# Second products of both tiles in one stretch, and earlier combinations of x and w, in a seven-product feed-forward kernel

## The chip, the cores and the metric

One core of one Trainium2 chip (trn2) runs the kernel. The metric is the device time in microseconds of one execution. The kernel before took 927.95 us (median of 3 runs, 927.69 to 928.31). A measurement of this kernel can tell about 0.2% (1.9 us) from no change.

## The reference

Three stages on 4 x 576 = 2304 tokens, all in float32:

```
scores = softmax(q k^T / 8) in chunks of 64 tokens, 8 heads of 64   # attention
x = scores v                                                        # 2304 x 512
y = ((x @ w_a) * (x @ w_b)) @ w_out                                 # 512 -> 1536 -> 512
h = y @ w_in;  g = P(h) / (Q(h) + 1e-6);  out = g @ w_out2          # 512 -> 2048 -> 512
```

P is a cubic with coefficients a, and Q = 1 + |b0||h| + |b1|h^2.

## The kernel before, in words

Every float32 product is made as three TensorE products of rounded halves (hi x hi, hi x lo, lo x hi). So each operand is first rounded to a "hi" part (a cast on ScalarE, `round_...`), and the rest is subtracted to a "lo" part (on GpSimd or VectorE, `rest_...`). All five engines run hand-written queues that meet at semaphores; an engine does its instructions strictly in the order in which they are written.

**Attention, merged with the first products.** 18 units of 128 tokens go through a pipeline (turns of 3 units), and between its steps TensorE does `merged_block`: the first two of twelve feature groups (`G1` = 2, the "first weights", cut into pieces by `FIRST_CUTS`) for five of the six tiles of 384 tokens. The sixth tile follows (`first1`, `second1(PLAIN)` and `second1(PLAIN + 1)`, L603 and L620).

**The quads.** The other ten feature groups of the middle stage are done two tiles at a time (3 pairs of tiles, 10 "quads" each, 30 in all). A quad n computes a 2 x 2 block product (two halves of the 512 inputs; the two tiles; the columns of w_a and w_b of one feature group) with seven products in place of eight. `quad_head(n)` (L649) does three of them, A11, S3 and S2; `quad_tail(n)` (L667) does A12, S1, A22 and S4. Each is 6 matmuls of 384 columns (`seven`, issued at L637). A11, A12 and A22 are blocks of the weights, S1 to S4 combinations that GpSimd makes (`sums`, L406), ScalarE rounds (`round_w`, L857) and GpSimd completes (`rest_ws`, L424). The other side needs combinations of x: T1, T2, T3 and T4, once per pair of tiles, of 128 x 768 each (`make_t1`, `make_t2`, `make_t4`, `round_t`, `rest_t`). GpSimd makes those of pair 0 during attention, VectorE those of pairs 1 and 2 between its other work.

**Around a quad.** ScalarE copies a product's bank as the seed of the next (`seed`, L926, which `quad_head` awaits before S2) and takes two partial results out (`copy_p7`, L931, and `copy_u2`, L936). VectorE's `corners(n)` (L1138 to L1145) adds and multiplies four times; the last matmuls of the quad, S4, wait for its first instruction (`c22_done`, L1138), which itself needs S1 to be done. The two results, one for each tile, are the gated values g of this feature group: ScalarE rounds them (`round_g`, L946), VectorE makes the rest (`rest_g`, L1150).

**A block** (`blk`, 15 in all) is quads 2 blk and 2 blk + 1, and between their parts the second products of the block before: `second_sum(blk - 1, ti)` for tile ti = 0 and 1, 24 matmuls each (L590), whose four banks VectorE adds to y (`add_y`, L1128). They need `wo_ready` (`round_wo`, L865, and `rest_wo`, L429). `round_g(n, ti)` waits for the `second_sum` of the same ti, since that still reads the older g. In block 0 there is no `second_sum`; `second1(PLAIN + 1)` of 12 matmuls (L626) stands in its place.

**Where weights lie.** `w` has four slots. Even quads use W_EVEN, odd ones W_ODD; the raw weights of even quads from 2 on come through a staging area. Part of the first weights lies in the columns S4 and up of W_ODD, so quad 1's combinations cannot be made before these are used up (`out_done`).

**The last stage** is 32 steps m of `first2(m)` (24 matmuls) and `second2(m - 3)` (18), with a rational function on ScalarE and VectorE in between. `second2(1)` needs the four pieces of its weights; the last piece is loaded after the last `second_sum`, rounded by ScalarE at step 3 (`round_w2(1, PPF2 - 1)`, L870) and completed by GpSimd (`rest_w2`, L434).

Of the kernel before, what the change touches and what calls it, by code (L numbers as in the profile page):

```python
# [20 lines left out]
def attention_moe_moe2(nc, q, k, v, w_a, w_b, w_out1, w_in, w_out2, a, b, out):  # L21
# [21 lines left out]
    PW = 512  # L43
# [41 lines left out]
    with ExitStack() as ctx:  # L85
# [118 lines left out]
        def first_w(half, start, n):  # L204
            if start < SLOT:
                assert start + n <= SLOT
                return w[:, T_ODD, half, start:start + n]
            return w[:, W_ODD, half, S4 + start - SLOT:S4 + start - SLOT + n]

        FIRST_CUTS = (0, PW, 2 * PW, 3 * PW, 4 * PW, SLOT, PPG1 * PW)  # L210
# [42 lines left out]
        LEAD_SPLIT = {2: (0, 1), 3: (2, 3), 4: (4, 5)}  # L253
        X2_AT = {2 * BPP: 0, 2 * BPP + 1: 1, 2 * BPP + 2: 2, 2 * BPP + 3: 3}

        def order_of_sums(n):
            return {0: 0, 1: 2, 2: 1}.get(n, n - 1 if n % 2 == 0 else n + 1 if n + 1 < QUADS else n)
# [31 lines left out]
        def _(sp):  # L289
# [53 lines left out]
            load_ab(0)  # L343
            load_wo(0)
            load_ab(1)
# [7 lines left out]
            load_wo(2)  # L353
            for blk in range(BLOCKS):
                if blk > 0:
                    sp.wait_ge(p3_done, 2 * blk)
                    load_ab(2 * blk + 1)
                    sp.wait_ge(sum_done1, DC * 2 * blk)
                else:
                    sp.wait_ge(out_done, G1)  # L360
                load_wo(2 * blk + 1)
                if 2 * blk + 4 < QUADS:
                    sp.wait_ge(ws_ready, 3 * (2 * blk + 3))
                    load_ab(2 * blk + 4)
                if 0 < blk < BLOCKS - 1:
                    sp.wait_ge(wo_ready, 2 * blk + 1)
                    load_wo(2 * blk + 2)
                if blk == 2 * BPP:
                    sp.wait_ge(p3_done, 2 * QPP)
                    for i in range(PPF2):  # L370
                        load_w2(0, i)
# [19 lines left out]
        def _(pool):  # L391
# [14 lines left out]
            def sums(n):  # L406

                pool.wait_ge(ab_loaded[n % 2], 32 * (n // 2 + 1))
                if n == 1:
                    pool.wait_ge(out_done, G1)  # L410
                half = lambda at: raw_w(n, at, at + HALF)
                nc.gpsimd.tensor_tensor(half(S1), half(S3), half(A22), ALU.add).then_inc(s1_done, 1)
                pool.wait_ge(s1_done, order_of_sums(n) + 1)
                nc.gpsimd.tensor_tensor(half(S2), half(S1), half(A11), ALU.subtract).then_inc(s2_done, 1)
                nc.gpsimd.tensor_tensor(half(S3), half(A11), half(S3), ALU.subtract).then_inc(sums_done, 1)
                pool.wait_ge(s2_done, order_of_sums(n) + 1)
                nc.gpsimd.tensor_tensor(half(S4), half(A12), half(S2), ALU.subtract).then_inc(sums_done, 1)
# [47 lines left out]
            for i in range(PPG1):  # L465
                rest_first(i)
# [34 lines left out]
        def _(pe):  # L501
# [186 lines left out]
            def merged_block(t, r, last=False):  # L688
# [12 lines left out]
                else:  # L701
                    pe.wait_ge(w_ready, PPG1)
# [100 lines left out]
        def _(act):  # L803
            def attention(turn, slot, stages):
                i = turn * RING + slot

                def split_first():
                    for n in LEAD_SPLIT.get(i, ()):
                        at, to = FIRST_CUTS[n], FIRST_CUTS[n + 1]
                        act.wait_ge(raw1_loaded[n], 16)  # L810
                        nc.scalar.copy(first_w(HI, at, to - at), y_flat[:, at:to]).then_inc(w_hi_done, 1)
# [47 lines left out]
            def round_wo(n):  # L859
                act.wait_ge(wo_loaded[n % 2], 16 * (n // 2 + 1))  # L860
                if n == 1:
                    act.wait_ge(out_done, G1)
                elif n >= 2:
                    act.wait_ge(sum_done1, DC * 2 * (n // 2))
                nc.scalar.copy(w[:, w_slot(n), HI, WO:SLOT], raw_w(n, WO, SLOT)).then_inc(wo_hi_done, 1)  # L865
# [6 lines left out]
            def round_t(pair, i):  # L872
                raw, hi, lo = t_parts(pair, i)
                act.wait_ge(t_made, T_MAKES * pair + (T_MAKES if i == T4 else 6))
# [82 lines left out]
            for blk in range(BLOCKS):  # L957
# [16 lines left out]
                round_w(n + 1, 1)  # L974
                round_w(n + 1, 2)
# [10 lines left out]
                if blk > 0:  # L986
                    round_wo(n)
# [17 lines left out]
            for m in range(STEPS2 + LAG2):  # L1005
# [50 lines left out]
        def _(dve):  # L1056
# [103 lines left out]
            def make_t1(pair):  # L1160
# [7 lines left out]
                nc.vector.tensor_tensor(t1, raw, x_block(x_hi, pair, 0, 0), ALU.subtract).then_inc(t_made, 1)  # L1168
                dve.wait_ge(t_made, made + 2)
                nc.vector.tensor_tensor(t1, t1, x_block(x_lo, pair, 0, 0), ALU.subtract).then_inc(t_made, 1)  # L1170

            def make_t2(pair):
                made, raw, (t1, t2, t4) = T_MAKES * pair, x_raw(pair), t_raw(pair)
                nc.vector.tensor_tensor(t4, x_block(x_hi, pair, 1, 1), x_block(x_lo, pair, 1, 1), ALU.add).then_inc(t_made, 1)
# [18 lines left out]
            for blk in range(BLOCKS):  # L1193
                n = 2 * blk
                if blk == 0:
# [4 lines left out]
                corners(n)  # L1200
# [4 lines left out]
                pair, part = blk // BPP + 1, blk % BPP  # L1205
# [97 lines left out]
```

## Time and profile before

| | |
|---|---|
| median of 3 runs | 927.95 us |
| the profiled execution, its own time | 927.83 us |
| its span | 926.1 us |
| TensorE busy | 903.2 us (98%) |
| VectorE busy | 676.3 us (73%) |
| ScalarE busy | 515.5 us (56%) |
| GpSimd busy | 361.4 us (39%) |
| mean granted TensorE clock | 0.996 of full |
| stages, from the chain of waits | attention to 158 us, quads to 512 us, last stage to the end |

The span is shorter than the time of the execution by 1.7 us, which lies around it. In the rows further on, a stretch is from:to in us from the span's start; a row of the chain is start, duration, engine, what it writes, line and how many instructions; a row of the timeline gives in brackets how long the engine had been idle before, and what released it.

### The profile page before, as it was taken

To read this page: it belongs to the slowest core of one execution; us is meant where nothing else is said; L and a number is where in the kernel's file an instruction comes from. 1 tells how busy PE (TensorE), PEld (TensorE's weight loads), DVE (VectorE), ACT (ScalarE), POOL (GpSimd) and SP (SyncE) were. 2 spreads that over 40 slices of the span, in tenths; PEclk is the share of its full clock that TensorE was granted. 3 is DMA by queue.
4 is the path that set the end of the run, shared out by engine and by line. 5 is a ranking of instruction groups with operands and counts; after the bars stand their busy time and mean duration, and the time that the engine had idled before them with its cause. 6 is when DMAs were issued, how large, how long until landed. Compare 5 with 4: busy or idle time off the path is not lost.

```text
span 926.1 us, 14075 instructions
## 1 busy us (share of the span) xinstructions
PE 903.2 (98%) x5596; PEld 852.7 (92%) x5596; DVE 676.3 (73%) x874; ACT 515.5 (56%) x786; POOL 361.4 (39%) x301
## 2 busy tenths in 40 slices
PE   8999999899899999999999989999999999999998
PEld 8899999899899999999999989999999999999996
DVE  3656552467655666665664798998999999989987
ACT  4655564333444445445553577776766666665662
POOL 2106133777867777778985223210111001100000
PEclk9999999999999999999999999999999999999999
DMA  9754611122122222123212020002000100000102
GB/s 212 165 104 103 137 24 35 58 69 65 49 69 69 69 69 58 51 73 106 84 53 73 20 91 1 1 1 91 0 1 1 57 35 1 1 1 22 48 35 102
DMA packets 103234, 53.35 MB, mean 58 GB/s; under 512 B 58880, under 2 KB 94720, under 8 KB 103168
## 3 DMA queue, kind: packets, MB, share of 16 engines
q1 hardware_dynamic: 103168, 52.45, 21.3%
q8 instruction: 44, 0.72, 0.3%
q14 instruction: 22, 0.18, 0.1%
HBM read 47.71 MB, written 4.72 MB: 57 GB/s over the span
## 4 chain that ended last, share of the span: by engine, by line
PE 90%; DVE 5%; issue 2%; ACT 1%; POOL 1%; DVEq 0%; ACTq 0%; POOLq 0%
PE ps L590 41%; PE ps L758 21%; PE ps L637 20%; PE ps L509 3%; PE ps L533 2%; PE ps L551 2%; PE ps L505 1%; DVE g_lo L1150 1%; POOL w L424 0%; PE ps L626 0%; DVE w L1168 0%; DVE w L1189 0%; DVE tmp L1138 0%; ACT g_hi L946 0%; DVE tmp L1247 0%
## 5 line engine op out<-in xcount | busy, mean ns | idle before, releaser
L590 PE MATMUL ps<-x_hi,w 128*128 128x384 f32 x960 | 255.3, 337 | 0.2 <-issue 0.2
L758 PE MATMUL ps<-w,g_hi 128*128 128x512 f32 x576 | 177.6, 391 | 2.6 <-POOL w L434 2.6
L590 PEld LDWEIGHTS ps<-x_hi,w 128*128 128x128 f32 x960 | 174.4, 188 | 2.9 <-issue 0.5
L590 PE MATMUL ps<-x_lo,w 128*128 128x384 f32 x480 | 160.8, 335 | 0.0
L590 PE MATMUL ps<-g_hi,w 128*128 128x384 f32 x560 | 148.7, 336 | 0.7 <-issue 0.7
L637 PE MATMUL ps<-x_hi,w 128*128 128x384 f32 x480 | 137.1, 341 | 11.8 <-DVE tmp L1138 8.1
L434 POOL TENSOR_TENSOR w<-w 128x512 fp32r<-128x512 f32 x32 | 46.9, 1470 | 240.5 <-ACT w L870 240.5
L758 PEld LDWEIGHTS ps<-w,g_hi 128*128 128x128 f32 x576 | 107.3, 188 | 23.9 <-POOL w L434 2.9
L758 PE MATMUL ps<-w,g_lo 128*128 128x512 f32 x288 | 112.1, 392 | 0.0
L1128 DVE TENSOR_TENSOR y<-y,ps 128x384 f32<-128x384 f32 x120 | 65.7, 553 | 59.5 <-PE ps L590 59.5
L637 PE MATMUL ps<-w 128*128 128x384 f32 x540 | 103.3, 334 | 0.0
L590 PEld LDWEIGHTS ps<-g_hi,w 128*128 128x128 f32 x560 | 101.7, 188 | 1.5 <-issue 1.1
L637 PEld LDWEIGHTS ps<-x_hi,w 128*128 128x128 f32 x480 | 89.7, 192 | 14.0 <-DVE tmp L1138 10.0
L946 ACT CAST g_hi<-tmp 128x384 fp32r<-128x384 f32 x60 | 30.8, 514 | 117.4 <-DVE tmp L1143 91.6
L637 PEld LDWEIGHTS ps<-w 128*128 128x128 f32 x540 | 94.6, 188 | 0.0
L590 PE MATMUL ps<-g_lo,w 128*128 128x384 f32 x280 | 93.6, 334 | 0.0
L590 PEld LDWEIGHTS ps<-x_lo,w 128*128 128x128 f32 x480 | 90.1, 188 | 1.7
L637 PE MATMUL ps<-x_lo,w 128*128 128x384 f32 x240 | 81.6, 340 | 0.0
L1030 ACT ACTIVATE w<-tmp,bias_ln 128x768 f32<-128x768 f32 x48 | 45.1, 940 | 60.5 <-DVE tmp L1253 60.3
L1013 ACT ACTIVATE tmp<-ps 128x768 f32<-128x768 f32 x48 | 39.0, 812 | 68.5 <-PE ps L590 68.5
L424 POOL TENSOR_TENSOR w<-w 128x512 fp32r<-128x512 f32 (+1 forms) x48 | 70.0, 1488 | 18.0 <-ACT w L857 16.8
L1247 DVE SCALAR_TENSOR_TENSOR tmp<-tmp,coef 128x768 f32<-128x768 f32 x48 | 53.3, 1110 | 30.2 <-ACT tmp L1016 30.1
(113 smaller groups left out, 1593.8 us busy)
## 6 DMA issues: line engine op xcount, KB each, us to landing
w<-in_moe_w_out SPq DMA_DIRECT2D x32, 256.0 KB, 3.5
out<-y SPq DMA_DIRECT2D x18, 256.0 KB, 2.0
y<-in_q SPq DMA_DIRECT2D x16, 256.0 KB, 4.3
y<-in_k SPq DMA_DIRECT2D x16, 256.0 KB, 4.5
y<-in_v SPq DMA_DIRECT2D x16, 256.0 KB, 3.3
w<-in_moe_w_a SPq DMA_DIRECT2D x16, 256.0 KB, 3.0
w<-in_moe_w_b SPq DMA_DIRECT2D x16, 256.0 KB, 3.4
w<-in_moe_w_in SPq DMA_DIRECT2D x16, 256.0 KB, 3.9
```

Source lines behind the costliest of these rows:

```text
L424: nc.gpsimd.tensor_tensor(w[:, w_slot(n), LO, at:to], raw_w(n, at, to), w[:, w_slot(n), HI, at:to], ALU.subtract).then_inc(ws_ready, 1)
L434: nc.gpsimd.tensor_tensor(w2_at(w, fp, LO, i), w2_at(w32, fp, LO, i), w2_at(w, fp, HI, i), ALU.subtract).then_inc(w2_ready, 1)
L509: last = nc.tensor.transpose(ps[:, bank, r * P:(r + 1) * P], x[:, r * P:(r + 1) * P], ident[:])
L533: last = nc.tensor.matmul(ps[rows, SC, at], qT[rows, at], kT[rows, at], start=True, stop=True)
L590: last = nc.tensor.matmul(dst, left, right, start=n == 0, stop=n == 3 * len(pairs) - 1)
L637: last = nc.tensor.matmul(ps[:, bank, 0:TILE], left, moving, start=i == 0 and not onto, stop=i == 5, skip_group_check=onto)
L758: last = nc.tensor.matmul(out_bank(n), left[:, 2 * (m % 2) + e, u * P:(u + 1) * P], w[:, slot2(fp), right, DC * HALF + e * D:DC * HALF + ( ...
L946: nc.scalar.copy(g_hi[:, 2 * ti + n % 2, :], corner[:, 2 * (n % 2) + 1 - ti, :]).then_inc(g_hi_done, 1)
L1013: nc.scalar.activation(habs, h, ACT.Abs).then_inc(habs_done, 1)
L1030: nc.scalar.activation(rec, den3[m % 2], ACT.Ln, scale=2.0 ** -SHIFT, bias=bias_ln[:, 0:1]).then_inc(ln_done, 1)
L1128: nc.vector.tensor_tensor(y[:, t, at], y[:, t, at], ps[:, 4 + c, 0:TILE], ALU.add).then_inc(y_added, 1)
L1247: nc.vector.scalar_tensor_tensor(out=den[cur], in0=den[cur], scalar=coef[:, 6:7], in1=habs, op0=ALU.add, op1=ALU.mult).then_inc(den_done, 1)
```

## The change

- **Order of a block on TensorE.** `quad_head(2 blk)` and `quad_tail(2 blk)` now follow each other, and `second_sum(blk - 1, 0)` and `second_sum(blk - 1, 1)` come behind them in one stretch (in block 0: `second1(PLAIN + 1)`). On VectorE `corners(2 blk)` goes ahead of `add_sums(blk - 1, 0)`.
- **Combinations of x for pairs 1 and 2** are spread over five blocks: two instructions behind `rest_g(n, 1)` in each, and the rests of T1 and T2 at the start of the blocks of parts 3 and 4. Before it was 3, 3, 4 and 2 instructions in the blocks of parts 1 to 4.
- **Quad 1's weights.** The first weights that lay in W_ODD from S4 on now lie in the WO columns of both W slots. So `sums(1)`, `round_w(1, ...)` and `rest_ws(1)` are done during attention, with earlier loads; in exchange the second weights of quads 0 and 1 (`load_wo`, `round_wo`, `rest_wo`) wait for `out_done` in block 0. A piece of the first weights is cut in two.
- **Pair 0** (T1 to T4) and quad 0's weights are rounded one step earlier in attention.
- **Last stage.** `round_w2(1, PPF2 - 1)` moves from the end of step 3 to the end of step 2 on ScalarE.

```diff
-            return w[:, W_ODD, half, S4 + start - SLOT:S4 + start - SLOT + n]
-        FIRST_CUTS = (0, PW, 2 * PW, 3 * PW, 4 * PW, SLOT, PPG1 * PW)
+            slot, at = (W_EVEN, W_ODD)[(start - SLOT) // D], WO + (start - SLOT) % D
+            assert at + n <= SLOT
+            return w[:, slot, half, at:at + n]
+        FIRST_CUTS = (0, PW, 2 * PW, 3 * PW, 4 * PW, SLOT, SLOT + D, PPG1 * PW)
...
@@ SyncE
-            load_ab(0)
-            load_wo(0)
-            load_ab(1)
+                if unit == 10:
+                    load_ab(0)
+                if unit == 12:
+                    load_ab(1)
...
-            load_wo(2)
             for blk in range(BLOCKS):
...
                 else:
                     sp.wait_ge(out_done, G1)
+                    load_wo(0)
                 load_wo(2 * blk + 1)
...
+                if blk == 0:
+                    sp.wait_ge(wo_hi_done, 1)
+                    load_wo(2)
@@ GpSimd
-                if n == 1:
-                    pool.wait_ge(out_done, G1)
...
             sums(0)
+            sums(1)
             for i in T_ORDER:
                 rest_t(0, i)
             rest_ws(0)
-            rest_wo(0)
+            rest_ws(1)
             sums(2)
             for blk in range(BLOCKS):
-                sums(2 * blk + 1)
-                rest_ws(2 * blk + 1)
+                if blk > 0:
+                    sums(2 * blk + 1)
+                    rest_ws(2 * blk + 1)
                 if blk < BLOCKS - 1:
                     rest_ws(2 * blk + 2)
-                if blk > 0:
-                    rest_wo(2 * blk)
+                rest_wo(2 * blk)
                 rest_wo(2 * blk + 1)
@@ TensorE
                 quad_head(2 * blk)
+                quad_tail(2 * blk)
                 if blk == 0:
                     second1(PLAIN + 1)
                 else:
                     second_sum(blk - 1, 0)
-                quad_tail(2 * blk)
-                if blk > 0:
                     second_sum(blk - 1, 1)
@@ ScalarE, attention
-                    if j == 1 and r == 4:
+                    if j == 1 and r == 3:
                         round_t(0, T1)
                         round_t(0, T2)
-                    if j == 1 and r == 5:
+                    if j == 1 and r == 4:
                         round_t(0, T3)
                         round_t(0, T4)
+                    if j == 1 and r == 5:
+                        round_w(0, 0)
+                        round_w(0, 1)
...
-                round_w(0, r)
-                if r == 2:
-                    round_wo(0)
+                if r == 0:
+                    round_w(0, 2)
+                round_w(1, r)
@@ ScalarE, blocks
-                round_w(n + 1, 0)
+                if blk > 0:
+                    round_w(n + 1, 0)
                 pair, part = blk // BPP + 1, blk % BPP
+                if pair < PAIRS and part == 2:
+                    round_t(pair, T1)
                 if pair < PAIRS and part == 3:
-                    round_t(pair, T1)
...
+                if m == 2:
+                    round_w2(1, PPF2 - 1)
                 if m == 3:
-                    round_w2(1, PPF2 - 1)
@@ VectorE
+                if pair < PAIRS:
+                    if part == 3:
+                        rest_t(pair, T1)
+                    if part == 4:
+                        rest_t(pair, T2)
+                corners(n)
                 if blk == 0:
                     for c in range(DC):
                         add_y(TILES - 1, -1, c)
                 else:
                     add_sums(blk - 1, 0)
-                corners(n)
                 rest_g(n, 0)
...
+                    if part == 0:
+                        make_t1_first(pair)
                     if part == 1:
-                        make_t1(pair)
+                        make_t1_last(pair)
                     if part == 2:
                         make_t2(pair)
                     if part == 3:
                         make_t4(pair)
-                        rest_t(pair, T1)
-                        rest_t(pair, T2)
```

The last instruction of `make_t1` and the first of `make_t2` are `make_t1_last`. Two places show how the instructions move.

VectorE in block 1, before, from `rest_g(2, 1)` to quad 3's first `corners` instruction (L1166 to L1170 are `make_t1` of pair 1):

```order
L1150 TENSOR_TENSOR g_lo<-tmp,g_hi 128x384 [waits g_hi_done]
L1166 TENSOR_TENSOR x_lo<-x_hi,x_lo 128x2x384 [waits out_done]
L1168 TENSOR_TENSOR w<-x_lo,x_hi 128x768 [waits t_made]
L1170 TENSOR_TENSOR w<-w,x_lo 128x768 [waits t_made]
L1138 TENSOR_TENSOR tmp<-ps,tmp 128x384 [waits p7_copied,p5_done]
```

The same engine after the change, from the end of quad 0's `corners` in block 0 to quad 1's first `corners` instruction (L1137 is `add_y`, L1161 `rest_g`, L1177 and L1179 `make_t1_first` of pair 1, L1149 the first of `corners`):

```order
L1156 TENSOR_TENSOR tmp<-ps,tmp 128x384 [waits p3_done]
L1137 COPY y<-ps 128x384 [waits out_done] x4
L1161 TENSOR_TENSOR g_lo<-tmp,g_hi 128x384 [waits g_hi_done] x2
L1177 TENSOR_TENSOR x_lo<-x_hi,x_lo 128x2x384 [waits out_done]
L1179 TENSOR_TENSOR w<-x_lo,x_hi 128x768 [waits t_made]
L1149 TENSOR_TENSOR tmp<-ps,tmp 128x384 [waits p7_copied,p5_done]
```

In block 1 one of the three instructions between `rest_g` and `corners` is gone; block 0, which had none there, has two.

ScalarE in block 0 after the change, from `copy_u2(0)` to `copy_u2(1)` (L954 is `round_g(0, ...)`, L862 `round_w(2, ...)`, L934 `seed(1)`, L870 `round_wo(0)`):

```order
L944 COPY tmp<-ps 128x384 [waits g_ready,p6_done]
L954 CAST g_hi<-tmp 128x384 [waits out_done,prod1_done]
L862 CAST w<-tmp 128x512 [waits p3_done,ab_loaded_even]
L862 CAST w<-tmp 128x512 [waits sums_done]
L862 CAST w<-tmp 128x768 [waits sums_done]
L954 CAST g_hi<-tmp 128x384 [waits out_done,prod2_done]
L934 COPY ps<-ps 128x384 [waits prod2_done,p1_done]
L870 CAST w<-w 128x512 [waits out_done,wo_loaded_even]
L939 COPY tmp<-ps 128x384 [waits g_ready,p7_done]
L944 COPY tmp<-ps 128x384 [waits g_ready,p6_done]
```

The three casts of quad 1's weights are gone from behind `copy_u2(0)`, and a cast of quad 0's second weights now stands between `seed(1)` and the copies of quad 1.

## Rows read from the trace of the kernel before

**Rows 1.** The page: busy times, and the chain that ended last by engine.

```profile
PE 903.2 (98%) x5596; PEld 852.7 (92%) x5596; DVE 676.3 (73%) x874; ACT 515.5 (56%) x786; POOL 361.4 (39%) x301
...
PE 90%; DVE 5%; issue 2%; ACT 1%; POOL 1%; DVEq 0%; ACTq 0%; POOLq 0%
```

**Rows 2.** Waits of TensorE: us in total, times, longest.

```profile
PE ps L637 <- DVE tmp L1138: 8.1, 6, 2.4
PE ps L637 <- POOL w L424: 3.7, 1, 3.7
PE ps L758 <- POOL w L434: 2.6, 1, 2.6
```

**Rows 3.** Stretches by block: length, busy PE, PEld, DVE, ACT, POOL; then clock.

```profile
158.18:183.46 25.28, 21.63 (x116) 21.31 (x115) 10.58 (x17) 9.72 (x19) 16.53 (x15) 0.93 0.17 52
183.46:207.59 24.13, 23.16 (x134) 22.84 (x133) 16.41 (x23) 9.63 (x18) 18.78 (x17) 1.00 0.24 67
...
231.72:258.81 27.09, 24.72 (x133) 24.40 (x133) 17.53 (x24) 11.83 (x21) 19.44 (x17) 0.94 0.22 60
258.81:281.69 22.88, 22.88 (x133) 22.88 (x133) 14.38 (x22) 10.27 (x19) 17.85 (x16) 1.00 0.22 64
...
352.83:377.83 25.00, 23.16 (x134) 22.84 (x133) 17.32 (x24) 11.84 (x21) 18.32 (x16) 1.00 0.26 72
```

**Rows 4.** The chain that ended last, in blocks 1 to 4.

```profile
202.56 0.56 DVE tmp L1138
...
203.16 4.43 PE ps L637 x24
...
252.82 5.99 PE ps L637 x24
...
271.29 10.40 PE ps L637 x60
```

**Rows 5.** Timeline of VectorE in block 1.

```profile
197.76 0.94 DVE L1166 TENSOR_TENSOR x_lo<-x_hi,x_lo 128x768 f32<-128x768 f32 x1
198.74 1.93 DVE L1168 TENSOR_TENSOR w<-x_lo,x_hi 128x768 f32<-128x768 f32 x1
```

**Rows 6.** Timeline of GpSimd in block 1.

```profile
193.07 4.35 POOL L424 TENSOR_TENSOR w<-tmp,w 128x512 fp32r<-128x512 f32 x3 [1.65 <-ACT w L857]
198.09 1.75 POOL L429 TENSOR_TENSOR w<-tmp,w 128x512 fp32r<-128x512 f32 x1 [0.67 <-ACT w L865]
```

**Rows 7.** The chain that ended last: block 0, and the start of the last stage.

```profile
166.54 4.61 POOL w L424 x3
...
171.20 12.26 PE ps L637 x60
...
548.38 4.38 PE ps L758 x18
```

**Rows 8.** Timeline of ScalarE in block 1.

```profile
192.38 1.88 ACT L857 CAST w<-tmp 128x512 fp32r<-128x512 f32 x3
...
197.02 0.46 ACT L926 COPY ps<-ps 128x384 f32<-128x384 f32 x1 [0.47 <-PE ps L637]
```

**Rows 9.** DMA issues by kind: KB each, median us from issue to landing.

```profile
w<-in_moe_w_out SPq DMA_DIRECT2D x32, 256.0 KB, 3.5
```

**Rows 10.** Timelines of GpSimd, TensorE and VectorE in the last stage.

```profile
546.79 1.53 POOL L434 TENSOR_TENSOR w<-w 128x512 fp32r<-128x512 f32 x1 [31.23 <-ACT w L870]
...
548.38 0.73 PE L758 MATMUL ps<-w,g_hi 128*128 128x512 f32 x2 [2.59 <-POOL w L434]
...
574.25 1.00 DVE L1266 SCALAR_TENSOR_TENSOR tmp<-tmp,coef,ps 128x768 f32<-128x768 f32 x1
```

**Rows 11.** Timelines of ScalarE and VectorE near the end of attention.

```profile
134.27 0.61 ACT L857 CAST w<-w 128x512 fp32r<-128x512 f32 x1
134.79 0.58 ACT L835 CAST x_hi<-ps 128x512 fp32r<-128x512 f32 x1
...
140.34 0.56 DVE L1100 TENSOR_TENSOR tmp<-ps,tmp 128x384 f32<-128x384 f32 x1 [0.37 <-ACT tmp L886]
```

More of the change, by code:

```diff
@@ L207, in first_w @@
                 return w[:, T_ODD, half, start:start + n]
-            return w[:, W_ODD, half, S4 + start - SLOT:S4 + start - SLOT + n]
-        FIRST_CUTS = (0, PW, 2 * PW, 3 * PW, 4 * PW, SLOT, PPG1 * PW)
+            slot, at = (W_EVEN, W_ODD)[(start - SLOT) // D], WO + (start - SLOT) % D
+            assert at + n <= SLOT
+            return w[:, slot, half, at:at + n]
+        FIRST_CUTS = (0, PW, 2 * PW, 3 * PW, 4 * PW, SLOT, SLOT + D, PPG1 * PW)
+        FIRSTS = len(FIRST_CUTS) - 1
         def w_slot(n):
@@ L250, in w2_at @@
             return tensor[:, slot2(fp), half, i * PW:(i + 1) * PW]
-        LEAD_SPLIT = {2: (0, 1), 3: (2, 3), 4: (4, 5)}
+        LEAD_SPLIT = {2: (0, 1), 3: (2, 3), 4: (4, 5, 6)}
         X2_AT = {2 * BPP: 0, 2 * BPP + 1: 1, 2 * BPP + 2: 2, 2 * BPP + 3: 3}
         def order_of_sums(n):
-            return {0: 0, 1: 2, 2: 1}.get(n, n - 1 if n % 2 == 0 else n + 1 if n + 1 < QUADS else n)
+            return {0: 0, 1: 1, 2: 2}.get(n, n - 1 if n % 2 == 0 else n + 1 if n + 1 < QUADS else n)
         def hidden(step):
@@ L463, in rest_t @@
                 nc.gpsimd.tensor_tensor(lo, raw, hi, ALU.subtract).then_inc(t_ready, 1)
-            for i in range(PPG1):
+            for i in range(FIRSTS):
                 rest_first(i)
@@ L701, in merged_block @@
                 else:
-                    pe.wait_ge(w_ready, PPG1)
+                    pe.wait_ge(w_ready, FIRSTS)
                     pe.wait_ge(g_ready, G1 * t + G1)
@@ L809, in split_first @@
                         at, to = FIRST_CUTS[n], FIRST_CUTS[n + 1]
-                        act.wait_ge(raw1_loaded[n], 16)
+                        act.wait_ge(raw1_loaded[min(n, PPG1 - 1)], 16)
                         nc.scalar.copy(first_w(HI, at, to - at), y_flat[:, at:to]).then_inc(w_hi_done, 1)
@@ L860, in round_wo @@
                 act.wait_ge(wo_loaded[n % 2], 16 * (n // 2 + 1))
-                if n == 1:
+                if n < 2:
                     act.wait_ge(out_done, G1)
-                elif n >= 2:
+                else:
                     act.wait_ge(sum_done1, DC * 2 * (n // 2))
@@ L873, in round_t @@
                 raw, hi, lo = t_parts(pair, i)
-                act.wait_ge(t_made, T_MAKES * pair + (T_MAKES if i == T4 else 6))
+                act.wait_ge(t_made, T_MAKES * pair + {T1: 3, T2: 6, T3: 6, T4: T_MAKES}[i])
                 nc.scalar.copy(hi, raw).then_inc(t_hi_done, 1)
@@ L973, in _ @@
                     round_t(pair, T4)
-                round_w(n + 1, 1)
-                round_w(n + 1, 2)
+                if blk > 0:
+                    round_w(n + 1, 1)
+                    round_w(n + 1, 2)
                 if blk in X2_AT:
@@ L985, in _ @@
                 seed(n + 1)
-                if blk > 0:
-                    round_wo(n)
+                round_wo(n)
                 copy_p7(n + 1)
@@ L1158, in rest_x2, with make_t1_first @@
                                         x_hi[:, :, tok], ALU.subtract).then_inc(x2_ready, 1)
-            def make_t1(pair):
+            def make_t1_first(pair):
                 made, raw, (t1, t2, t4) = T_MAKES * pair, x_raw(pair), t_raw(pair)
@@ L1168, in make_t1, with make_t1_last @@
                 nc.vector.tensor_tensor(t1, raw, x_block(x_hi, pair, 0, 0), ALU.subtract).then_inc(t_made, 1)
+            def make_t1_last(pair):
+                made, raw, (t1, t2, t4) = T_MAKES * pair, x_raw(pair), t_raw(pair)
                 dve.wait_ge(t_made, made + 2)
                 nc.vector.tensor_tensor(t1, t1, x_block(x_lo, pair, 0, 0), ALU.subtract).then_inc(t_made, 1)
+                nc.vector.tensor_tensor(t4, x_block(x_hi, pair, 1, 1), x_block(x_lo, pair, 1, 1), ALU.add).then_inc(t_made, 1)
             def make_t2(pair):
                 made, raw, (t1, t2, t4) = T_MAKES * pair, x_raw(pair), t_raw(pair)
-                nc.vector.tensor_tensor(t4, x_block(x_hi, pair, 1, 1), x_block(x_lo, pair, 1, 1), ALU.add).then_inc(t_made, 1)
                 dve.wait_ge(t_made, made + 4)
@@ L1194, in _ @@
                 n = 2 * blk
+                pair, part = blk // BPP + 1, blk % BPP
+                if pair < PAIRS:
[4 more added lines that the diff above has]
+                corners(n)
                 if blk == 0:
@@ L1204, in _ @@
                 rest_g(n, 1)
-                pair, part = blk // BPP + 1, blk % BPP
                 if pair < PAIRS:
+                    if part == 0:
+                        make_t1_first(pair)
                     if part == 1:
-                        make_t1(pair)
+                        make_t1_last(pair)
                     if part == 2:
```

## The prediction, made before the changed kernel ran

> **What bounds the kernel now.** I read the page first: TensorE is busy in 98% of the span and makes up 90% of the chain that ended last, VectorE 5% [rows 1]. So only places where TensorE stands still can be won, and no engine beside it matters unless it makes TensorE wait. Then the waits of TensorE, which name those places: six times behind VectorE's L1138 (8.1 us, the longest 2.4), once behind GpSimd's L424 (3.7), once behind GpSimd's L434 (2.6) [rows 2]. The third view is the quads cut into blocks, from one first `second_sum` to the next. A block without a stall is 132 matmuls in 22.88 us [rows 3], 0.1733 us each; a product of 6 is 1.04 us, a quad 7.28, a `second_sum` 4.16. Against that, the first row (158.18:183.46) has 114 matmuls, worth 19.76 us, and takes 25.28; the block from 231.72 takes 27.09, the one from 352.83 takes 25.00, and four take 24.13 (the one from 183.46 stands for all four) [rows 3].
>
> **Term 1, combinations of x on VectorE.** The six slow blocks are those of parts 1 to 3 of pairs 1 and 2. Between `rest_g(n, 1)` and `corners(n + 1)` VectorE does three or four instructions of 768 columns there. In block 1 TensorE ends the second `second_sum` at 195.95 (183.46 and three stretches of 4.16) and could start S4 6.24 us later, at 202.19; L1138 would have to start by 201.63, but it starts at 202.56, and TensorE resumes at 203.16 with 24 matmuls in 4.43 instead of 4.16 us, so a restart costs 0.27 [rows 4]. After the change at most two such instructions stand there. The first two of block 1 end at 200.7 (198.74 + 1.93) [rows 5], 0.9 us before the limit, and GpSimd's and ScalarE's work at that place is the same in each block. What remains is late nowhere, so all six blocks become 22.88: 4 x 1.25 + 4.21 + 2.12 = **11.3 us gained**. The instructions that move to the start of the blocks of parts 3 and 4 (one each, 0.94 alone, 1.93 at worst) have room: `rest_g` of the quad before ends about 2.6 us into the block, and `corners(n)` is wanted at 5.2.
>
> **Term 2, block 0.** Now TensorE waits 3.7 us for quad 1's weights, which GpSimd ends at 171.15, and the first matmuls after it run at the lower clock: 60 in 12.26 where 60 elsewhere take 10.40 [rows 4, 7]; the stretch has a mean granted clock of 0.93, a mix of the two levels, 1.2 and 2.4 GHz [rows 3]. In the change these weights are ready before the quads begin. But two other waits come. Count from 158.18, the start of quad 0. Quad 0 ends at 7.28, `second1` at 9.36, S2 of quad 1 could start at 11.44. ScalarE begins `round_g(0, 0)` at 9.42, then does three casts (1.88 us) [rows 8], `round_g(0, 1)` and only then `seed(1)`, of 0.46 us [rows 8]: overlaps taken off, it ends at 12.55, and TensorE resumes at 12.60, a stall of **1.16**. S1 then ends at 15.99 and S4 could start at 17.03. VectorE meanwhile has `add_y` (to 11.35), two `rest_g` and the two new instructions, all with both inputs in SBUF, while GpSimd runs `rest_ws(2)` from 10.5 (three instructions, 4.35 us) [rows 6] and then `rest_wo(0)`, whose weights land about 3.5 us after 9.4 [rows 9].
>
> How such instructions meet decides the term. L1166 of 768 columns takes 0.94, and L1168, of the same size, 1.93, while GpSimd's L429 runs from 198.09 for 1.75 rather than its usual 1.28 [rows 5, 6]: each seems to wait until the other's instruction has ended, in turn. Played forward so, `rest_g` ends at 12.3 and 14.0, GpSimd's third at 15.8, the first new instruction at 16.7, `rest_wo(0)` at 17.9, the second new one at 18.8, and L1138 at 19.3. TensorE stalls **2.3 us** more, and quad 1 ends at 20.68 where it now ends at 22.16. I let the load of these weights cost nothing beside this, since ScalarE's cast of them (13.0 to 13.6) ends before S2 does. Whether the clock falls again is open: after 2.4 us of waiting 24 matmuls took 5.99 instead of 4.43 [rows 4], after 2.59 us 18 of the last stage took 4.38 instead of 4.12, a bare restart [rows 7, 10], after 3.7 they slowed. With two stalls in 7 us I take the fall, 1.6 us. So block 0 **loses 0.1 us**; without the fall it gains 1.5, and without the second stall 4.1.
>
> The Trainium skill, "SBUF — State Buffer", section "Who interferes with whom", says that a VectorE instruction with two SBUF inputs and a GpSimd instruction that reads SBUF exclude each other for the whole instruction, whoever issues first. By that rule block 0 is the loss of 0.1 (or the gain of 1.5) above; by the durations of the same instructions undisturbed it would be the gain of 4.1. The trace agrees with the page so far: 1.93 beside 0.94 [rows 5].
>
> **Term 3, last stage.** GpSimd completes the last piece of the weights from 546.79, right behind ScalarE's cast, and TensorE goes on at 548.38 after 2.59 us [rows 10], which with the restart is 2.85. One step earlier the cast would run at 539.5, and the wait is gone. But VectorE and ScalarE run their own chain there, delayed by their own long work, and TensorE now only meets it later: `first2(8)` starts at 577.68 now (548.38, 4.38 for `second2(1)`, three steps of 8.3), would start at 574.83, and needs L1266 of step 6, which ends at 575.25 [rows 10] and moves by about +0.1. That gives back 0.5 and a restart. **2.0 us gained**, between 1.0 and 2.85.
>
> **Term 4, attention.** ScalarE has one cast of 768 and one of 512 in front of `round_x` where one of 512 stands at 134.27; `round_x` starts the moment that cast ends [rows 11]. So it comes 0.75 later, and VectorE's chain behind it reaches L1100 at 140.76 instead of 140.34, which TensorE waits for: 0.4. With the casts at the step before, where two delay it by 0.1 now, I take **0.5 lost**, between 0.2 and 1.5. The combination of quads 0 and 1 moves to 84 to 90 us on GpSimd, beside one VectorE instruction that has 1 us to spare, and the cut piece adds one ScalarE instruction before 32 us, also covered.
>
> **Nothing** for `second_sum` in one stretch: each bank of the second is wanted 4.16 us after the first wrote it, and `add_y` takes 0.55 of every 1.04. Nothing either for quad tails right behind heads: odd quads run so already, 60 matmuls without a gap in 10.40 [rows 4]. If the cover went, the price would be that of the rival below.
>
> **Sum.** 927.83 (the profiled execution's own time, 0.1 below the median) - 11.3 + 0.1 - 2.0 + 0.5 = **915.1 us**.
>
> **Rivals.**
> 1. *VectorE and GpSimd do not hold each other up in block 0, or the clock stays up.* For it: the 2.59 us wait that slowed nothing. Against it: L1168. 927.8 - 11.3 - 4.1 - 2.0 + 0.5 = 910.9 without the second stall; 913.5 with it at full clock. Chance 0.34 together, most of it for 913.5.
> 2. *The two instructions left are still late in some blocks*, because GpSimd's L429 now falls behind each of them. Each of up to ten blocks would then lose what passes the margin of 0.9 us, some 0.4 and the restart of 0.27: up to 7 us given back, 922. Against it: in part 4 of pair 1 two such instructions stand there now, and the block from 258.81 takes 22.88 [rows 3]. Chance 0.08.
> 3. *Slower: even quads begin to wait.* Their tail now follows at once, so L1138 is wanted by 5.68 us into a block, where it had until 9.8. Ahead of it stand the last of `corners`, two `rest_g` and ScalarE's `seed` and `round_g`. 14 blocks times a stall s must exceed 12.7: it decides from s = 0.9, that is L1138 starting at 6.6 instead of 5.2. At 1.2 the time is 932. Against it: odd quads have the same order and no stall. Chance 0.06, a third of it about the break-even.
> 4. *The change doesn't do what it says*: quad 1's weights, or the loads moved into attention, come late and a new wait of 3.7 us and more stands at quad 0. Then 919 to 920. Against it: TensorE never waits for quad 0's weights or a load now [rows 2], and the new ones come by the same queues. Chance 0.04.
>
> **The numbers.** 0.48 for my forecast of 915.1, the rest as above. The range of 910.9 to 918.8 takes in rival 1, the bounds of terms 2 to 4, and a small part of rival 2; less than 0.2 is left out. A measurement of this kernel can tell 0.2% (1.9 us) from no change; every case but rival 3 is faster by more: faster 0.94, same 0.02, slower 0.04.
>
> **What would show it.** In the changed profile: all blocks from block 1 on at 22.88 us; no wait behind the first `corners` instruction but one in block 0, of 2.3 us; a wait of about 1.2 behind `seed` there; lower clock in the quads once at most; no wait behind GpSimd at the start of the last stage, and a short one some 29 us into it. I am wrong if a block after block 0 is longer than 23, or if block 0 is under 22 us up to quad 2's end of head.

## The result and the profile after

The changed kernel takes **914.18 us** (median of 4 runs, 911.74 to 914.71; the kernel before, timed four times beside it, 927.82): a ratio of 0.9847, 95% interval 0.9829 to 0.9866. The forecast was 915.1, the range 910.9 to 918.8. The profiled execution is the fastest of the four, 911.74 us, with a span of 910.0.

The waits of TensorE, to be read against [rows 2] (the functions moved by some lines: L643 is `seven`, L1149 the first of `corners`, L934 `seed`, L596 `second_sum`, `first2` and the first products). Two short ones of attention and the one of 2.5 us at the very start are left out:

```profile
PE ps L643 <- DVE tmp L1149: 1.8, 1, 1.8
PE ps L596 <- issue: 1.2, 2, 1.0
PE ps L643 <- ACT ps L934: 1.1, 1, 1.1
...
PE ps L596 <- DVE tmp L1285: 0.3, 1, 0.3
```

The second line is a wait near the end of attention and a shorter one at the start of the last stage; in the kernel before it was

```profile
PE ps L590 <- issue: 1.0, 2, 0.7
```

Six waits behind `corners` have become one, the wait for quad 1's weights and the one for the last piece of the last stage are gone, and two new ones are there, behind `seed` (1.1) and behind VectorE in the last stage (0.3). The wait near the end of attention has grown from 0.7 to 1.0. That the earlier loads and casts removed the wait for quad 1's weights is read from this list; no run undoes that part.

The stretches of the quads, as in [rows 3], cut from the start of quad 0 and then from one first `second_sum` to the next:

```profile
157.75:185.18 27.43, 24.51 (x140) 23.87 (x139) 16.61 (x22) 9.73 (x20) 15.43 (x14) 1.00 0.23 68
185.18:208.05 22.87, 22.87 (x133) 22.87 (x133) 14.86 (x23) 10.40 (x20) 17.68 (x17) 1.00 0.24 70
208.05:230.93 22.88, 22.88 (x134) 22.88 (x133) 15.75 (x24) 11.17 (x21) 17.71 (x17) 1.00 0.25 69
230.93:253.81 22.88, 22.88 (x134) 22.88 (x133) 15.46 (x24) 9.98 (x19) 17.22 (x16) 1.00 0.25 70
345.31:368.19 22.88, 22.88 (x134) 22.88 (x133) 15.72 (x24) 10.55 (x20) 18.19 (x17) 1.00 0.24 69
```

Every block behind block 0 takes 22.88, to 0.02, those of parts 1 to 3 too. Only the first stretch has TensorE standing still: 24.51 busy of 27.43. Its chain shows where:

```profile
157.75 7.28 PE ps L643 x42
165.03 2.09 PE ps L632 x12
...
167.15 1.95 DVE y L1137 x4
169.10 2.48 DVE g_lo L1161 x2
171.59 2.53 DVE x_lo L1177
...
174.14 0.03 DVE w L1179
...
175.99 0.56 DVE tmp L1149
...
176.59 8.59 PE ps L643 x48
```

Quad 0, `second1`, then not TensorE but VectorE's queue: `add_y`, two `rest_g`, the two new instructions, and L1149, which TensorE waits for. The `seed` stall lies inside this stretch, hidden by the longer one. By stage, in the profiled executions: attention 158.18 to 157.75 us, the quads 354.06 to 340.71 (498.46 less 157.75), the last stage 413.86 to 411.54.

### The profile page after: what moved, and what is told of

The parts are those of the page before. It is cut to its first block, busy times and chain, and to the rows that moved or that the text cites. A ratio compares the mean times of both kernels' runs of the same rounds, so it can differ in the third digit from the quotient of the medians.

```text
span 910.0 us, 14077 instructions
## 1 busy us (share of the span) xinstructions
PE 898.0 (99%) x5596; PEld 848.7 (93%) x5596; DVE 676.6 (74%) x874; ACT 515.1 (57%) x787; POOL 356.7 (39%) x302
## 4 chain that ended last, share of the span: by engine, by line
PE 92%; DVE 4%; ACT 2%; issue 1%; POOL 0%; DVEq 0%; ACTq 0%; POOLq 0%
PE ps L596 40%; PE ps L643 23%; PE ps L764 19%; PE ps L515 3%; PE ps L539 2%; PE ps L557 2%; PE ps L511 1%; DVE tmp L1266 1%; DVE tmp L1272 1%; ACT w L1040 1%; PE ps L632 0%; ACT g_hi L1053 0%; ACT tmp L1026 0%; ACT tmp L1023 0%; DVE tmp L1262 0%
## 5 line engine op out<-in xcount | busy, mean ns | idle before, releaser
L596 PE MATMUL ps<-x_hi,w 128*128 128x384 f32 x960 | 255.4, 337 | 0.6 <-DVE tmp L1285 0.3
L596 PEld LDWEIGHTS ps<-x_hi,w 128*128 128x128 f32 x960 | 174.4, 188 | 3.6 <-DVE tmp L1285 0.7
L596 PE MATMUL ps<-x_lo,w 128*128 128x384 f32 x480 | 160.8, 335 | 0.0
L596 PE MATMUL ps<-g_hi,w 128*128 128x384 f32 x560 | 146.5, 336 | 1.0 <-issue 1.0
L643 PE MATMUL ps<-x_hi,w 128*128 128x384 f32 x480 | 134.2, 334 | 1.8 <-DVE tmp L1149 1.8
L643 PE MATMUL ps<-w 128*128 128x384 f32 x540 | 103.4, 334 | 1.1 <-ACT ps L934 1.1
L596 PEld LDWEIGHTS ps<-g_hi,w 128*128 128x128 f32 x560 | 101.5, 188 | 1.8 <-issue 1.4
L954 ACT CAST g_hi<-tmp 128x384 fp32r<-128x384 f32 x60 | 30.9, 515 | 118.5 <-PE ps L596 63.6
L643 PEld LDWEIGHTS ps<-w 128*128 128x128 f32 x540 | 94.4, 188 | 1.5 <-ACT ps L934 1.5
L596 PE MATMUL ps<-g_lo,w 128*128 128x384 f32 x280 | 93.6, 334 | 0.0
L596 PEld LDWEIGHTS ps<-x_lo,w 128*128 128x128 f32 x480 | 90.1, 188 | 1.7
L643 PEld LDWEIGHTS ps<-x_hi,w 128*128 128x128 f32 x480 | 87.8, 188 | 2.1 <-DVE tmp L1149 2.1
L643 PE MATMUL ps<-x_lo,w 128*128 128x384 f32 x240 | 80.2, 334 | 0.0
```

Of the source, the lines that this page charges most:

```text
L596: last = nc.tensor.matmul(dst, left, right, start=n == 0, stop=n == 3 * len(pairs) - 1)
L643: last = nc.tensor.matmul(ps[:, bank, 0:TILE], left, moving, start=i == 0 and not onto, stop=i == 5, skip_group_check=onto)
L954: nc.scalar.copy(g_hi[:, 2 * ti + n % 2, :], corner[:, 2 * (n % 2) + 1 - ti, :]).then_inc(g_hi_done, 1)
```

## The experiments

All are edits of the changed kernel. Two lengths serve to compare them: the median, and in the profile the time from quad 0 to the last stage ("the quads", 340.71 in the changed kernel), which leaves attention and the start out. The kernel before, timed beside each set of runs, took 927.82, 928.13, 928.76 and 928.65 us, so medians of different sets compare to about 1 us only, and the quads' length is the surer measure.

### Where executions of the changed kernel differ

The same kernel again (`changed_again`).

> The changed kernel, unaltered, to see where its executions differ (911.7 to 914.7 us). Theory A (mine): TensorE's granted clock. In the profiled execution of 911.7 it never fell in block 0, in the longer ones it falls behind the two stalls there (1.1 and 1.8 us), which costs about 1.6, and the first transposes of the start take 4.95 us instead of 4.09. So a profiled execution of 914 us shows block 0 some 1.6 us longer, and nothing else in the quads. Rival B: the loads or VectorE's waits differ from run to run; then a stretch behind block 0 is longer, at full clock.

Measured: 913.02 us (4 runs, 911.62 to 914.19); the profiled execution took 914.03. The chain at the start of the kernel, then in block 0:

```profile
2.49 4.95 PE ps L511 x22
...
176.66 0.56 DVE tmp L1149
177.22 0.04 issue
177.26 10.16 PE ps L643 x48
```

48 matmuls in 10.16 where the faster execution has 8.59 behind the same wait of 1.8: 1.57 us. Stretches of this execution:

```profile
158.44:187.42 28.98, 26.06 (x139) 25.42 (x139) 15.98 (x22) 10.67 (x21) 16.76 (x15) 0.94 0.22 64
177.20:181.00 3.80, 3.74 (x14) 3.74 (x15) 2.16 (x5) 0.89 (x3) 2.92 (x4) 0.65 0.53 170
```

The granted clock is 0.65 on average just behind the stall, a mix of 1.2 and 2.4 GHz. The start has 4.95 instead of 4.09 us for 22 transposes, of which 0.69 is left when the quads begin (158.44 against 157.75). The two make 2.26 of the 2.29 between 914.03 and 911.74. Theory A holds for the quads: the spread there is the clock behind block 0's stalls. The mean granted clock of each execution says the same: 1.000 in the three that took 911.6 to 912.0 us, 0.998 in the five that took 914.0 to 914.7. For the start it is not shown: the granted clock over these transposes reads 1.00 in both profiles, so why they take 0.86 us longer in one stays open.

### The order of a block on TensorE undone

```diff
                 quad_head(2 * blk)
-                quad_tail(2 * blk)
                 if blk == 0:
                     second1(PLAIN + 1)
                 else:
                     second_sum(blk - 1, 0)
+                quad_tail(2 * blk)
+                if blk > 0:
                     second_sum(blk - 1, 1)
```

and `corners(n)` behind `add_y` again on VectorE, in all blocks.

> The order of the block undone in all 15 blocks, on TensorE and VectorE (second product of tile 0 back between head and tail of the even quad, add_y ahead of corners); all else as changed. Theory A: the two stalls of block 0 come from ScalarE's queue ahead of seed(1) and from VectorE's and GpSimd's instructions ahead of the first corners instruction, and both are the same in either order, since round_g(0, 0) waits for quad 0's product, done 9.4 us into the block both ways; the later blocks have slack in both orders. So 914.2, within 0.7. Rival B: putting the second products behind the quad is what hides VectorE's work; then blocks 1 to 14 are longer than 22.88 and the time is 918 or more. Rival C: the new order causes block 0's stalls; then 910 to 911.

Measured: 911.46 us (911.21 to 911.85), the quads 340.47. Its waits:

```profile
PE ps L643 <- DVE tmp L1150: 1.5, 1, 1.5
...
PE ps L643 <- ACT ps L935: 1.2, 1, 1.2
```

The two stalls of block 0 are there in the old order as well, 1.2 and 1.5 us, so rival C falls; the later blocks are no longer than with the new order, so rival B falls. By the profiles at full clock the two orders differ by 0.24 us. The median is 2.7 below that of the changed kernel's first four runs and 1.6 below the second four: none of the four executions here has the fall of the clock (the mean granted clock is 1.000 in each), which theory A missed (I expected 914.2 within 0.7). Whether the shorter stall (1.5 for 1.8) is why, four runs don't show. What they do show: the part of the change that names it, the second products in one stretch, brings nothing by itself.

### The spread of the x combinations undone

`make_t1`, `make_t2`, `make_t4` and the rests back in the blocks of parts 1 to 4, and the cast of T1 back in part 3.

> The combinations of x for pairs 1 and 2 back in the blocks of parts 1 to 4 (3, 3, 4 and 2 instructions, casts as before), all else as changed. Theory A: the six stalls return, 1.25 four times, 4.2 and 2.1, in all 11.3, and block 0 loses its second stall (2.06 and the fall of the clock there): 914.2 + 11.3 - 2.1 less up to 1.5, that is 922 to 923.5. Rival B: with the second products in one stretch the longer groups are hidden: under 918.

Measured: 922.55 us (920.82 to 923.22), the quads 349.94. From its waits, and then the parts of its chain on TensorE, from block 1 to the start of block 4:

```profile
PE ps L643 <- DVE tmp L1148: 8.0, 6, 2.3
```

```profile
182.96 8.33 PE ps L596 x48
...
198.76 8.59 PE ps L643 x48
207.35 8.33 PE ps L596 x48
...
222.82 8.59 PE ps L643 x48
231.41 8.33 PE ps L596 x48
...
248.28 10.03 PE ps L643 x48
258.31 8.32 PE ps L596 x48
```

The six waits are back, 8.0 us as before, with blocks of 24.39, 24.06 and 26.90 us. Without the second stall of block 0 (1.79 and 0.27) the changed kernel's quads would be 338.65; 349.94 is 11.3 more. That is term 1, measured; 1.4 of it is the fall of the clock in block 3 (48 matmuls in 10.03 for 8.59), which the kernel before had at the same place (27.09 in [rows 3]).

### Block 0: the seed first

```diff
                 round_g(n, 0)
+                if blk == 0:
+                    seed(n + 1)
                 if blk < BLOCKS - 1:
                     for i in range(3):
                         round_w(n + 2, i)
                 round_g(n, 1)
-                seed(n + 1)
+                if blk > 0:
+                    seed(n + 1)
```

> In block 0 alone, ScalarE does seed(1) right behind round_g(0, 0), ahead of the three casts of quad 2's weights. Theory A: the stall behind seed (1.1 us) goes, but quad 1's S4 still waits for VectorE's chain, which now starts later since GpSimd's three rests start about 0.9 later; by instructions that wait for each other in turn the first corners instruction comes 0.5 to 1.5 us later, as one stall of 3 to 4 us. So no gain: 914.5 to 916. Rival B: a stall removed is time gained: 1.4 us less, 912.8.

Measured: 915.49 us (912.75 to 917.02), the quads 342.96. Two of TensorE's waits, then a piece of the chain in block 0 (L1152 is the first of `corners`, L944 `copy_u2`):

```profile
PE ps L643 <- DVE tmp L1152: 2.8, 1, 2.8
...
PE ps L643 <- ACT tmp L944: 0.9, 1, 0.9
```

```profile
180.35 10.07 PE ps L643 x48
```

The wait behind `seed` is gone; one of 0.9 behind `copy_u2` and one of 2.8 behind `corners` stand in its place, and the clock falls (10.07 for 48). Without that fall the quads would be 341.48, still 0.8 longer than the changed kernel's. A stall in front of a later and longer one is worth nothing. The time of 917.02 of this profiled execution has one more cause, which the edit does not explain: in attention, at 29 us, TensorE waits 2.2 us where the changed kernel waits 0.8, and the clock falls behind it (0.83 on average from 28 to 38 us), so that quad 0 starts at 160.75 instead of 157.75. What it waits for the profile does not show. So the quads, not the median, carry this reading.

### Block 0: the two combinations behind the quad

```diff
-                    if part == 0:
+                    if part == 0 and blk > 0:
                         make_t1_first(pair)
...
                 corners(n + 1)
                 rest_g(n + 1, 0)
                 rest_g(n + 1, 1)
+                if blk == 0:
+                    make_t1_first(pair)
```

> In block 0 alone, VectorE makes the first two instructions of pair 1's combinations behind rest_g(1, 1) instead of ahead of corners(1). Theory A: these two, held up by GpSimd, are the second stall; it goes (1.79 and 0.27 for the restart), no new one comes, and with one stall of 1.1 us left the clock no longer falls in block 0. So 2.1 less than the changed kernel at equal clock and up to 3.6 less in the median: 910.5 to 912. Rival B: another wait (the copies of quad 1, or quad 1's weights) stands right behind it: within 0.5 of 914.2.

Measured: 910.39 us (910.25 to 912.34), the quads 339.34: 1.4 shorter than the changed kernel at full clock, not 2.06. Two of its waits:

```profile
PE ps L643 <- ACT ps L934: 1.1, 1, 1.1
...
PE ps L643 <- DVE tmp L1149: 0.4, 1, 0.4
```

The wait of 1.8 is gone; the one of 0.4 stands in block 1, where GpSimd's rests now meet the next two combinations (the first takes 2.59 us instead of 0.95) and VectorE's `corners` comes just too late. With the seed first on top:

> Both edits of block 0 together: seed(1) ahead of the casts, and pair 1's first two instructions behind corners(1). Theory A: with VectorE's chain out of the way the seed stall is worth its 1.14 + 0.27 too, so block 0 runs without a stall: 1.4 below the kernel with the second edit alone, 909 to 910.5. Rival B: the casts, now later, delay GpSimd's rests of quad 2 or round_g, and TensorE waits at quad 2 instead: no better than the second edit alone.

Measured: 911.17 us (910.94 to 911.33), the quads 339.23. A miss: the 1.1 behind `seed` turned into 0.9 behind `copy_u2` (ScalarE's casts now stand in front of the copies), and block 1's stall grew to 0.6. Rival B, with a place I had not named.

### Do the instructions of VectorE and GpSimd exclude each other?

```diff
-                rest_wo(2 * blk)
-                rest_wo(2 * blk + 1)
+                if blk > 0:
+                    rest_wo(2 * blk)
+                    rest_wo(2 * blk + 1)
                 if 2 * blk + 4 < QUADS:
                     sums(2 * blk + 4)
+                if blk == 0:
+                    rest_wo(0)
+                    rest_wo(1)
```

> In block 0 alone, GpSimd does rest_wo(0) and rest_wo(1) behind sums(4), which wait for a load until 178.1, so GpSimd is idle from 173.3 to then. Theory A (exclusive instructions): VectorE's second new instruction, L1179, is no longer held up and takes 0.94 instead of 1.92; the first corners instruction starts 0.9 to 1.0 us earlier and the stall falls from 1.8 to about 0.85: 913.2, or 911.7 where the clock then stays up. Rival B: L1179 is slow by its own operands: it still takes 1.9 and the time stays at 914.2.

Measured: 911.90 us (911.84 to 912.35). VectorE and GpSimd in the changed kernel:

```profile
171.51 2.60 DVE L1177 TENSOR_TENSOR x_lo<-x_hi,x_lo 128x768 f32<-128x768 f32 x1
174.14 1.92 DVE L1179 TENSOR_TENSOR w<-x_lo,x_hi 128x768 f32<-128x768 f32 x1
...
168.32 4.97 POOL L429 TENSOR_TENSOR w<-tmp,w 128x512 fp32r<-128x512 f32 x3 [14.89 <-ACT w L862]
173.25 3.95 POOL L434 TENSOR_TENSOR w<-w 128x512 fp32r<-128x512 f32 x2
```

and in this one (L1183 is the same instruction as L1179):

```profile
171.94 2.60 DVE L1181 TENSOR_TENSOR x_lo<-x_hi,x_lo 128x768 f32<-128x768 f32 x1
174.58 0.96 DVE L1183 TENSOR_TENSOR w<-x_lo,x_hi 128x768 f32<-128x768 f32 x1
...
168.75 4.97 POOL L429 TENSOR_TENSOR w<-tmp,w 128x512 fp32r<-128x512 f32 x3 [14.89 <-ACT w L866]
177.85 0.74 POOL L417 TENSOR_TENSOR tmp<-tmp 128x256 f32<-128x256 f32 x1 [4.13 <-DMA tmp<-in_moe_w_b]
```

The first is unchanged, 2.60 where it takes 0.94 alone, since GpSimd's third rest holds it (here to 173.72, that is 168.75 + 4.97). The second takes 0.96 instead of 1.92 with GpSimd idle, on the same operands. TensorE's wait there falls from 1.8 to 0.9 us, as theory A had it. At full clock little is won by it: block 0 is 0.97 shorter (26.46 for 27.43), block 1, where GpSimd is now late, 0.46 longer (23.34), and the quads are 340.35 for 340.71. The lower median goes with a clock that falls in none of the four executions (1.000 in each). The rule of the Trainium skill, "SBUF — State Buffer", section "Who interferes with whom", as weighed in the prediction, is borne out: 0.96 against 1.92.

### The last piece of the weights in its old place

```diff
-                if m == 2:
-                    round_w2(1, PPF2 - 1)
                 if m == 3:
+                    round_w2(1, PPF2 - 1)
```

> ScalarE rounds the last piece of the second weights of step 1 at the end of step 3 again, as before. Theory A: the wait of 2.6 us returns at the start of the last stage and the shorter one behind L1285 (0.3 and a restart) goes: 2.3 more, 916.5. Rival B: the whole stage is bound by VectorE's chain there, and it makes no difference: 914.2 to 914.7.

Measured: 916.56 us (915.48 to 918.27), 2.4 more than the changed kernel. In its chain, and then its timeline of TensorE:

```profile
535.64 1.54 POOL w L439
537.23 5.96 PE ps L764 x18
```

```profile
537.23 1.15 PE L764 MATMUL ps<-w,g_hi 128*128 128x512 f32 x2 [2.59 <-POOL w L439]
```

The wait is the same 2.59 us as before [rows 10], but here 18 matmuls behind it take 5.96 us instead of 4.38 [rows 7]. The last stage of this execution is 415.40 us against 411.54; 1.58 of the 3.86 is the clock, 2.28 the wait net of the shorter one behind L1285, which is gone.

### A better version

ScalarE waits 5.8 us in block 0 before `round_g(0, 0)`, while the casts behind it need only quad 0. With the new order on TensorE quad 0 is done 2.1 us before `out_done`; in the old one it is done only behind it.

```diff
                 copy_p7(n)
                 copy_u2(n)
+                if blk == 0:
+                    for i in range(3):
+                        round_w(n + 2, i)
...
-                if blk < BLOCKS - 1:
+                if 0 < blk < BLOCKS - 1:
                     for i in range(3):
                         round_w(n + 2, i)
...
-                round_wo(n)
+                if blk > 0:
+                    round_wo(n)
                 copy_p7(n + 1)
                 copy_u2(n + 1)
+                if blk == 0:
+                    round_wo(n)
```

> In block 0 alone, ScalarE does the three casts of quad 2's weights right behind copy_u2(0), where it is idle for 5.8 us (they need only quad 0 to be done, 2.1 us before out_done), and round_wo(0) behind copy_u2(1). Theory A: the seed stall goes (1.14 + 0.27); GpSimd's rests of quad 2 end about 2 us earlier, so the first corners instruction of quad 1 starts at about 16.0 us into the block where S4 could start at 15.6: the stall of 1.8 shrinks to about 1. Quads 2.3 shorter at equal clock (338.4 us from quad 0 to the last stage, where the changed kernel has 340.7), no fall of the clock, time 909 to 910.5. Rival B: quad 1's copies or the weights of the second product become late: a new stall of 0.5 to 1 in block 0 or 1, 911 as with seed_first_and_t1_after.

Measured: 910.48 us (5 runs, 909.25 to 910.87), the quads 338.78, and one wait left in them:

```profile
PE ps L643 <- DVE tmp L1155: 1.0, 1, 1.0
```

It stands behind `corners` in block 0. The stall behind `seed` is gone and the other is 1.0, as theory A had it; the time is at the upper end of its range and the quads are 0.4 longer than the 338.4 expected. With `rest_wo` later in addition:

> The same, and GpSimd's rest_wo(0) and rest_wo(1) behind sums(4) in block 0. Theory A: nothing holds L1179's counterpart up any more; the first corners instruction is in time and block 0 has no stall: 3.5 less in block 0, but up to 0.8 given back in block 1, where GpSimd comes about 1 us late (as in rest_wo_later). Quads 337.3 to 338.0, time 908.5 to 909.5. Rival B: block 1 gives all of it back: 910 or more.

Measured: 910.34 us (909.90 to 910.90), the quads 338.69. Block 0 has no wait left, but block 1 has one of 0.8: a miss of 0.7 us, rival B. With quad 0's third cast one step earlier in attention:

> The same, and quad 0's third cast moved from the end of attention to the step before, behind its other two. Theory A: TensorE's wait near the end of attention for VectorE's chain behind round_x shrinks from 1.0 to 0.7 as in the kernel before, and nothing else changes: 0.3 less than the kernel of the run before this one, 908.2 to 909.2. Rival B: three casts in one step (1.9 us) delay that step's own chain, and it is the same or worse.

Measured: **909.61 us** (909.39 to 910.56; 0.9794 of the kernel before, interval 0.9778 to 0.9810). The wait near the end of attention is 0.7 again, as in the kernel before:

```profile
PE ps L600 <- issue: 1.0, 2, 0.7
```

That is the 0.3 that was expected (quad 0 starts at 158.36 instead of 158.70). The time is a miss all the same, 0.4 above the range, since the version it builds on had already missed its own (910.34 for at most 909.5). And another 0.7 came unasked: the quads are 337.96 instead of 338.69, because the wait of 0.8 in block 1 is all but gone. In block 1 the two queues meet otherwise (GpSimd starts its first rest 2.05 us into the block, for 1.56); one profile of each kernel does not show that the moved cast is the reason, so this part is luck as far as is known. In the chain one stall of under 0.1 us is left in the quads, in block 1 (197.32 where 197.23 was possible):

```profile
158.36 7.28 PE ps L647 x42
...
174.04 8.61 PE ps L647 x48
182.66 8.33 PE ps L600 x48
...
194.75 1.50 DVE w L1194
...
197.32 8.59 PE ps L647 x48
205.92 8.32 PE ps L600 x48
```

It beats both kernels: 4.6 below the changed kernel's 914.18, 3.4 below its second median, and its interval of ratios lies below both of theirs (0.9829 to 0.9866, 0.9818 to 0.9851). At full clock the quads are 2.75 shorter (337.96 for 340.71); the rest goes with a clock that no longer falls.

## Why the prediction was right, point by point

- **Term 1**, 11.3 us: right. All six slow blocks are at 22.88, and with the old spread 11.3 come back.
- **Term 2**, 0.1 lost, or 1.5 won with the clock up. The places were right: behind `seed` 1.14 (forecast 1.16), behind `corners` 1.79 (2.3). Quad 1 ends 20.15 us after the start of quad 0 (185.18 less quad 2's 7.28, less 157.75), where 20.68 was forecast and 22.16 stood before: the second stall was over-sized by 0.5, since VectorE's chain, played forward, ran that much faster on the chip: `rest_g` ended at 13.83 us from the start of quad 0 for 14.0, the first new instruction at 16.36 for 16.7, the second at 18.31 for 18.8. Block 0 wins 2.0 at full clock and 0.4 with the fall. The fall of the clock is real but not the rule: of two profiled executions of this kernel one shows it and one does not, and by their granted clock it came in five of eight. The case that I took is the commoner one, but only just; that the median of the first four stands beside my forecast is in that part luck.
- **Term 3**, 2.0 won: 2.3. The wait is gone and the short one is there, 0.3 and a restart, where 0.5 and a restart were forecast; it stands at `first2(8)`, at 561 us, as forecast.
- **Term 4**, 0.5 lost: about 0.3 (the wait near the end of attention is 1.0 for 0.7, and the last version wins that back). That attention ends 0.43 earlier in the profiled execution is the start: 4.09 us for the first 22 transposes in place of 4.95.
- **Nothing** for the second products in one stretch: right, 0.24 us at full clock, and the wrong way.
- **Rivals.** Of 1, the half with the second stall at full clock (913.5) is what three of the eight executions are, at 911.6 to 912.0; the half without the second stall did not come, and the run with `rest_wo` later shows that VectorE and GpSimd do hold each other up. 2 did not come in this kernel (it did, with up to 0.8 us, in block 1 of the variants that changed when GpSimd comes). 3 and 4 did not come.
- **Sum.** For the profiled execution: 927.83 - 11.3 - 2.0 - 2.3 + 0.3 and - 0.7 for the start give 911.8, measured 911.74. For the executions with the fall, my 915.1 less what was mis-sized (0.5 in block 0, 0.3 in the last stage, 0.2 in attention) is 914.1; they took 914.0 to 914.7.

## What to carry to other kernels

A stall's price is read at the last wait behind it, not at its own: removing the first of two stalls in one quad won nothing while the second queue ended later; moving the work ahead of both to where its engine was idle won 1.9 of the 3.5 us that the two cost with their restarts, and 2.75 in the last version. When work is spread to avoid six stalls, count the instructions at each place against the time until the next engine wants something, with each instruction of VectorE on two SBUF operands lengthened by GpSimd's instruction beside it. And the name of a change need not be the part that pays: undoing the order alone cost nothing, undoing the spread cost 8 us and more.

## What the runs showed of the hardware

The granted clock after a stall of TensorE is not fixed by the stall's length. The same wait of 1.8 us in the same place is followed by 48 matmuls in 8.59 us in one execution and 10.16 in another; the same wait of 2.59 us by 18 matmuls in 4.38 and in 5.96. Each fall costs 1.4 to 1.6 us. But the length matters: the changed kernel, with a stall of 1.8 us in the quads, has a mean granted clock of 0.998 in five of eight executions, while the seven versions whose longest stall in the quads is 1.5 us or less have 0.999 or 1.000 in all 29. So the changed kernel spreads over 3 us; the versions whose longest stall in the quads is 1.1 us or less spread over 0.4 to 1.6, and one over 2.1 by a single run. At the start the first 22 transposes take 4.09 to 4.96 us from one execution to the next at a granted clock that reads 1.00 throughout; no run shows why.

An instruction of VectorE on two SBUF operands and one of GpSimd wait for each other's end, in turn: VectorE's L1179 of 768 columns takes 1.92 us beside GpSimd and 0.96 with it idle, GpSimd's L434 of 512 columns beside it 2.0 us and elsewhere 1.28. A stretch of matmuls behind a wait takes 0.27 us more than without one (48 in 8.59 for 8.32), beside the wait itself.
